# Two half-filled matmuls of the first layers issued as a pair on the two row halves of TensorE

## The reference

```python
# attention: batch 4, 8 heads, 768 steps, head size 40; q, k, v, three gates
for t in range(S):
    m_new = maximum(f[t] + m, i[t])
    C = exp(f[t] + m - m_new) * C + exp(i[t] - m_new) * outer(v[t], k[t])
    n = exp(f[t] + m - m_new) * n + exp(i[t] - m_new) * k[t]
    y[t] = sigmoid(o[t]) * (C @ q[t]) / maximum(abs(n . q[t]), 1)
x = y.transpose(0, 2, 1, 3).reshape(3072, 320)
# first MLP
h = x @ w_in            # 320 -> 2048
x = maximum(0.01 * h, h) @ w_out      # 2048 -> 320
# second MLP, weights of its own
h = x @ w2_in
out = (h * cos(h)) @ w2_out
```

## Time and profile before

| | |
|---|---|
| median of 3 executions | 838.56 us (837.67 to 840.02) |
| the profiled execution | 840.17 us, span 838.4 us |
| TensorE matmuls busy | 818.4 us, 98% of the span, 6939 matmuls |
| VectorE, ScalarE, GpSimd busy | 76%, 55%, 41% |
| mean granted TensorE clock | 0.989 of full speed |
| first MLP with attention of the next blocks | from about 37 us to 477 us |
| second MLP | from about 477 us to the end |

### The profile page before, as it was taken

The page is one execution under the profiler, slowest core; times in us unless marked ns, Lnnn a source line. Parts: engine busy times, 40 slices in busy tenths (PEclk is TensorE's granted clock), DMA queues, the critical chain, the costliest instruction groups (busy, mean ns, idle before and its releaser), DMA issues.

```text
span 838.4 us, 18237 instructions
## 1 busy us (share of the span) xinstructions
PE 818.4 (98%) x6939; PEld 787.9 (94%) x6939; DVE 636.8 (76%) x1377; ACT 465.1 (55%) x1033; POOL 339.6 (41%) x350
## 2 busy tenths in 40 slices
PE   8789999999999999999999999999999999999997
PEld 6679899999999999999999999999999999999997
DVE  7778678677677776777754488888888888888886
ACT  5245343433443434334436687767677767777776
POOL 5755634344333333443315643333333333333332
PEclk9989999999999999999999999999999999999999
DMA  8494433322334333226023320302020202020000
GB/s 262 130 249 129 151 84 93 125 78 80 125 104 128 124 81 125 78 78 194 2 90 100 106 102 2 118 2 72 1 72 1 72 1 71 1 72 1 17 8 25
DMA packets 37292, 70.26 MB, mean 84 GB/s; under 512 B 3544, under 2 KB 24408, under 8 KB 37208
## 3 DMA queue, kind: packets, MB, share of 16 engines
q1 hardware_dynamic: 36708, 68.86, 26.5%
q10 hardware_dynamic: 500, 0.26, 0.1%
HBM read 57.11 MB, written 11.99 MB: 82 GB/s over the span
## 4 chain that ended last, share of the span: by engine, by line
PE 90%; DVE 5%; ACT 2%; DMA 1%; issue 1%; SPq 1%; POOL 1%; DVEq 0%; POOLq 0%; ACTq 0%
PE h L621 31%; PE acc L633 13%; PE acc L635 13%; PE acc L634 12%; PE s L621 10%; PE x L599 2%; PE s L579 2%; PE s L563 2%; PE s L591 2%; PE s L544 1%; DMA raw_out<-w1o 1%; DVE g_lo L1180 1%; DVE C L1161 1%; DVE t_f L1037 1%; DMA e_dram<-r_f 0%
## 5 line engine op out<-in xcount | busy, mean ns | idle before, releaser
L621 PE MATMUL h<-xT,w_in 128*128 128x384 f32 x1536 | 307.8, 342 | 0.7 <-DVE xT L1172 0.7
L621 PEld LDWEIGHTS h<-xT,w_in 128*128 128x128 f32 x1536 | 267.8, 189 | 3.8 <-DVE xT L1172 0.9
L777 ACT ACTIVATE t_f<-h 128x384 f32<-128x384 f32 x192 | 94.1, 490 | 294.5 <-PE h L621 294.4
L633 PE MATMUL acc<-w_out,g_hi 128*128 128x320 f32 x768 | 242.7, 316 | 2.1 <-POOL g_lo L1519 1.7
L635 PE MATMUL acc<-w_out,g_lo 128*128 128x320 f32 x768 | 237.9, 310 | 0.0
L634 PE MATMUL acc<-w_out,g_hi 128*128 128x320 f32 x768 | 236.7, 308 | 0.0
L1519 POOL TENSOR_TENSOR g_lo<-g_f,g_hi 128x384 fp32r<-128x384 f32 x127 | 130.0, 1023 | 212.1 <-ACT g_hi L777 212.1
L1193 DVE TENSOR_TENSOR g_f<-h,t_f 128x384 f32<-128x384 f32 x128 | 71.2, 556 | 109.2 <-ACT t_f L777 109.1
L633 PEld LDWEIGHTS acc<-w_out,g_hi 128*128 128x128 f32 x768 | 144.9, 189 | 4.6 <-POOL g_lo L1519 1.9
L634 PEld LDWEIGHTS acc<-w_out,g_hi 128*128 128x128 f32 x768 | 145.1, 189 | 0.0
L635 PEld LDWEIGHTS acc<-w_out,g_lo 128*128 128x128 f32 x768 | 144.7, 188 | 0.0
(11 more groups left out here) (150 smaller groups left out, 797.6 us busy)
## 6 DMA issues: line engine op xcount, KB each, us to landing
qk_s<-qk SPq DMA_DIRECT2D x24, 512.0 KB, 3.8
kvo_s<-kvo SPq DMA_DIRECT2D x24, 484.0 KB, 5.2
x_dram<-stage SPq DMA_DIRECT2D x8, 960.0 KB, 5.5
xT<-x_dram SPq DMA_DIRECT2D x8, 960.0 KB, 4.9
D<-g_dram SPq DMA_DIRECT2D x42, 128.0 KB
qe<-q SPq DMA_DIRECT2D x24, 160.0 KB, 5.5
out<-x SPq DMA_DIRECT2D x24, 160.0 KB, 1.8
eG_b<-e_dram SPq DMA_DIRECT2D x42, 80.0 KB
```

The source lines that it names most:

```text
L621: last = nc.tensor.matmul(bank[:, 0:BLOCK], w(a), x[:, k, :], start=(n == 0), stop=(n == 7))
L633: nc.tensor.matmul(acc[t][:, 0:DM], g_hi[:, s, r], w_out[:, 0, j, :], start=(j == 0), stop=False)
L777: copy = lambda o, i, **k: nc.scalar.activation(o, i, ACT.Copy, **k)
```

## The change

`w_in` loses chunk 5. Chunk 2 now holds, for an even tile, the high part of the rest in rows 0 to 63 and its low part in rows 64 to 127; for an odd tile the two are swapped (`rest_rows`). `xT` and `stage` gain chunk 5: chunk 2 holds the rest's high part in both halves, chunk 5 its low part in both. Matmul (2, 2) gives high times high and low times high. What is left, high times low, has 64 rows. It is one matmul of 64 rows for each tile, on rows 0 to 63 for an even tile and on rows 64 to 127 for an odd one (`rest_product`). Both are issued behind the seven full ones of the even tile, one behind the other, into two banks. So an even slot has 7 full matmuls and the pair, an odd slot 7 full ones. The wait for the odd tile's bank moves from its slot into the even slot, ahead of the second of the pair. `split_turned` is one instruction of 128 x 384 instead of two. The low parts of the weights are written in two or three instructions instead of one, on GpSimd with a wait between them. The tokens' DRAM buffer grows from 5 to 6 chunks.

```diff
-        w_in = sb("w_in", [P, 6, FF], F32R)
+        w_in = sb("w_in", [P, 5, FF], F32R)
-        xT = sb("xT", [P, 2, 5, BLOCK], F32R)
-        stage_f = sb("stage", [P, 5, BLOCK])
+        xT = sb("xT", [P, 2, 6, BLOCK], F32R)
+        stage_f = sb("stage", [P, 6, BLOCK])
...
+        def rest_rows(j):
+            return slice(SUB * (1 - j % 2), SUB * (2 - j % 2))
...
             def first_product(bank, x, j):
                 w = lambda k: w_in[:, k, j * P:(j + 1) * P]
-                order = [(0, 0), (0, 3), (3, 0), (1, 1), (1, 4), (4, 1), (2, 2), (5, 2)]
+                order = [(0, 0), (0, 3), (3, 0), (1, 1), (1, 4), (4, 1), (2, 2)]
                 for n, (a, k) in enumerate(order):
-                    last = nc.tensor.matmul(bank[:, 0:BLOCK], w(a), x[:, k, :], start=(n == 0), stop=(n == 7))
+                    last = nc.tensor.matmul(bank[:, 0:BLOCK], w(a), x[:, k, :], start=(n == 0 and j % 2 == 0),
+                                            stop=(n == 6 and j % 2 == 1))
+                if j % 2 == 0:
+                    last = rest_product(bank, x, j)
                 last.then_inc(h_done, 1)
+
+            def rest_product(bank, x, j):
+                r = side(j % 2)
+                return nc.tensor.matmul(bank[:, 0:BLOCK], w_in[r, 2, j * P:(j + 1) * P], x[r, 5, :], start=(j % 2 == 1), stop=(j % 2 == 0))
...
-                    pe.wait_ge(max_done, row.tile(i) - 1 + H_FREE)
+                    if j % 2 == 0:
+                        pe.wait_ge(max_done, row.tile(i) - 1 + H_FREE)
                     first_product(h_bank[i % 2], xT[:, row.half(i)], j)
+                    if j % 2 == 0:
+                        pe.wait_ge(max_done, row.tile(i) + H_FREE)
+                        rest_product(h_bank[1], xT[:, row.half(i)], j + 1)
                 elif exists(row, i):
...
-                    pe.wait_ge(prod_done, row.tile2(i) - 3 + PROD_FREE)
+                    if j % 2 == 0:
...
+                        pe.wait_ge(prod_done, row.tile2(i) - 3 + PROD_FREE)
                     first_product(ring_bank[i % 4], xT[:, row.half(i)], j)
+                    if j % 2 == 0:
...
+                        pe.wait_ge(prod_done, row.tile2(i) - 2 + PROD_FREE)
+                        rest_product(ring_bank[(i + 1) % 4], xT[:, row.half(i)], j + 1)
...
-                tt(dst[:, 3:5, r], src[:, 0:2, :], dst[:, 0:2, r].bitcast(F32), ALU.subtract)
-                return tt(dst[REM:P, 2, r], src[REM:P, 2, :], dst[REM:P, 2, r].bitcast(F32), ALU.subtract)
+                return tt(dst[:, 3:6, r], src, dst[:, 0:3, r].bitcast(F32), ALU.subtract)
...
 (VectorE, six pieces of two tiles)
-                tt(w_in[:, 3:6, c], raw_in[:, k % RAW_IN, :, :], w_in[:, 0:3, c].bitcast(F32), ALU.subtract).then_inc(win_lo, 1)
+                for j in range(PT):
+                    r, b = rest_rows(j), slice((k * PT + j) * P, (k * PT + j + 1) * P)
+                    tt(w_in[r, 2, b], raw_in[r, k % RAW_IN, 2, j * P:(j + 1) * P], w_in[r, 2, b].bitcast(F32), ALU.subtract)
+                tt(w_in[:, 3:5, c], raw_in[:, k % RAW_IN, 0:2, :], w_in[:, 0:2, c].bitcast(F32), ALU.subtract).then_inc(win_lo, 1)
...
 (GpSimd, two pieces; the second MLP's tiles likewise, in two instructions)
-                nc.gpsimd.tensor_tensor(w_in[:, 3:6, c], raw_in[:, k % RAW_IN, :, :], w_in[:, 0:3, c].bitcast(F32),
-                                        ALU.subtract).then_inc(win_lo, 1)
+                nc.gpsimd.tensor_tensor(w_in[:, 3:5, c], raw_in[:, k % RAW_IN, 0:2, :], w_in[:, 0:2, c].bitcast(F32),
+                                        ALU.subtract).then_inc(win_step, 1)
+                pool.wait_ge(win_step, PT * k + 1)
+                for j in range(PT):
+                    r, b = rest_rows(j), slice((k * PT + j) * P, (k * PT + j + 1) * P)
+                    nc.gpsimd.tensor_tensor(w_in[r, 2, b], raw_in[r, k % RAW_IN, 2, j * P:(j + 1) * P], w_in[r, 2, b].bitcast(F32),
+                                            ALU.subtract).then_inc(win_step if j == 0 else win_lo, 1)
+                    if j == 0:
+                        pool.wait_ge(win_step, PT * k + 2)
...
-    x2_dram = nc.dram_tensor("x2_dram", [BLOCKS, P, 5, BLOCK], F32, kind="Internal").ap()
+    x2_dram = nc.dram_tensor("x2_dram", [BLOCKS, P, 6, BLOCK], F32, kind="Internal").ap()
```

More of the change, by code:

```diff
@@ L164, in build @@
         win_lo = sem("win_lo")
+        win_step = sem("win_step")
         wout_hi = sem("wout_hi")
@@ L661, in slot @@
                         pe.wait_ge(x2_in[row.half(i)], row.block(i) * 8 - 8 * row.half(i) - 48)
[L662 to L665, removed]
-                    pe.wait_ge(prod_done, row.tile2(i) - 3 + PROD_FREE)
-                    first_product(ring_bank[i % 4], xT[:, row.half(i)], j)
+                    if j % 2 == 0:
+                        if row.starts(BLOCKS, i):
+                            pe.wait_ge(win_lo, PIECES + j + 2)
+                            if j == 0:
+                                pe.wait_ge(max_done, row.tile(i) - 1 + H_FREE)
+                        pe.wait_ge(prod_done, row.tile2(i) - 3 + PROD_FREE)
+                    first_product(ring_bank[i % 4], xT[:, row.half(i)], j)
+                    if j % 2 == 0:
+                        if row.starts(BLOCKS, i) and j == 0:
+                            pe.wait_ge(max_done, row.tile(i) + H_FREE)
+                        pe.wait_ge(prod_done, row.tile2(i) - 2 + PROD_FREE)
+                        rest_product(ring_bank[(i + 1) % 4], xT[:, row.half(i)], j + 1)
                 if (u := row.unit(i, TURN)) and j < FT - 1:
@@ L1455, in swap_in_lo @@
                 k, c = PIECES + j // PT, slice(j * P, (j + 1) * P)
-                nc.gpsimd.tensor_tensor(w_in[:, 3:6, c], raw_in[:, k % RAW_IN, :, j % PT * P:(j % PT + 1) * P],
-                                        w_in[:, 0:3, c].bitcast(F32), ALU.subtract).then_inc(win_lo, 1)
+                r, b = rest_rows(j), slice(j % PT * P, (j % PT + 1) * P)
+                nc.gpsimd.tensor_tensor(w_in[:, 3:5, c], raw_in[:, k % RAW_IN, 0:2, b], w_in[:, 0:2, c].bitcast(F32),
+                                        ALU.subtract).then_inc(win_step, 1)
+                pool.wait_ge(win_step, PT * RAW_IN + j + 1)
+                nc.gpsimd.tensor_tensor(w_in[r, 2, c], raw_in[r, k % RAW_IN, 2, b], w_in[r, 2, c].bitcast(F32),
+                                        ALU.subtract).then_inc(win_lo, 1)
+                pool.wait_ge(win_lo, PIECES + j + 1)
             def swap_out_lo(j):
```

## The result

| | before | after |
|---|---|---|
| median of 4 runs each, same chip | 838.13 us (837.67 to 840.02) | 864.36 us (862.51 to 864.64) |
| ratio | | 1.0306, 95% interval 1.0285 to 1.0328 |
| the profiled execution | 840.17 us, span 838.4 | 864.11 us, span 862.4 |
| TensorE matmuls busy | 818.4 us | 840.1 us |
| VectorE busy | 636.8 us | 635.7 us |

The account below looks back on a forecast made before the run. TensorE was taken to bound the kernel, with 90% of the chain. Pairs' net +28.8 us, shared switches -2.4 and first block -0.5 gave +25.9 on 838.56, so 864.5 us; range 858 to 871, widened to 854 to 873.

Parts of the forecast that it names:

- The step that decides: TensorE entering and leaving the 64-row shape costs 0.40 us a pair, against 0.175 gained by running side by side.
- Rivals 1 to 3: Shape change free or cheap (816 us if free, chance 0.06); half price (0.09); pair not side by side (887 us, 0.05).
- rival 2: Half the switch price, for instance if entry's cost hangs on a semaphore wait: 842 or 839 us; chance 0.09.
- What the profile was to show: Second MLP: two slots 5.68 us, entry 0.27, second layer's first matmul 0.35; TensorE 90% or more; VectorE's busy time falls.
- The net of a pair: Switch cost less matmul time saved: +0.225 us for each of 128 pairs, +28.8 us.
- The shared switch: Blocks 1 to 6, slots 0 and 10: scores follow, so the pair adds one shape change, 12 times 0.20, -2.4 us.
- The moved waits: Waits for the odd tile's bank, moved forward, cost nothing: 1.25 us to spare in first MLP, 2.5 in second.
- VectorE's and GpSimd's edits: Weight splits and units' low parts: hidden, priced at nothing; uncovered, up to 2 us in the first block.
- DMA: Tokens' buffer a fifth larger: landings of at most 6.6 and 5.9 us, loaded a block ahead, cost nothing.
- The forecast's own range: 858 to 871 us for switches of 0.36 to 0.45 us a pair, chance 0.80; widened to 854 to 873.
- the first block's bounds: First block's 8 pairs: -0.5 us taken for hidden ones, bounds -1.8 (all hidden) and +3 (low clock, other edits showing).
- The total: Whole kernel: +28.8 - 2.4 - 0.5 = +25.9 us, median to 864.5 us, 3.1% slower.

Follow-up runs that it names:

- e3: Changed kernel without the pair's second matmul (odd tiles lack high times low of the rest), waits as before the change: 864.76 us, ratio 1.0311.
- e4: Changed kernel with both matmuls of the pair on rows 0 to 63: 884.56 us, ratio 1.0534.
- e1: Changed kernel with its other edits, but one full 128-row matmul per tile instead of the pair and waits where they were: 842.91 us, ratio 1.0032.
- e8: e1 with 93 tiles of the second MLP run wholly in 64-row halves, both layers, upper halves not added up: 839.72 us, ratio 0.9994.
- e6: Changed kernel with 80 instead of 128 stationary columns in both matmuls of the pair: 858.14 us, ratio 1.022.
- e2: e1 with the eighth matmul of odd tiles left out, so 15 full matmuls for two tiles and no pair: 822.22 us, ratio 0.9801.
- e5: e1 with 18 pairs only, in blocks 1 to 6, straight behind the state unit: 840.48 us, ratio 1.0013.
- e7: Changed kernel with 64 instead of 384 moving columns in both matmuls of the pair: 848.61 us, ratio 1.0099.
- v1: Kernel before, with the low part of the rest in six first-block weight pieces moved from VectorE to GpSimd: 841.45 us, ratio 1.003.
- e10: e1 without the twelve small VectorE instructions writing the rest's low part for the first MLP's tiles 4 to 15: 834.93 us, ratio 0.9959.

## Why the prediction was right, point by point

**The step that decides: right.** Forecast: 0.09 at entry, 0.11 for the pair's first load, 0.09 and 0.11 at the exit. Found: 0.095 ahead of the pair, 0.194 between it and the second layer (its load and the drain), 0.104 ahead of that layer's second matmul (its first load); 0.396 against 0.40. That it runs side by side: e3 and e4. That it is the shape and nothing else: e1 at 0.00 in steady blocks, and e8 paying 0.38 to 0.41 where full and halved layers meet. That the load is in the open: e6. Rivals 1 to 3 are out; rival 2 since the entry has its gap though the pair's first matmul waits for no semaphore.

**What the profile was to show.** 5.68 us for two slots (5.66), 0.27 (0.27), a duration longer by 0.11 (0.44 against 0.34), 0.35 for the second layer's first matmul (0.34). Two signs were off: TensorE has 88% of the chain and not 90% or more, and VectorE's busy time fell by 1.1 us where I had 4 to 5. The units' low parts gave their 7 us and the weights' took 3 more than before. Most of the rest is a subtraction that the change doesn't touch, that of `g_lo`, before and after:

```profile
L1180 DVE TENSOR_TENSOR g_lo<-g_f,g_hi 128x384 fp32r<-128x384 f32 x128 | 95.3, 744 | 0.0
```

```profile
L1202 DVE TENSOR_TENSOR g_lo<-g_f,g_hi 128x384 fp32r<-128x384 f32 x128 | 100.1, 782 | 0.0
```

Its 128 instructions took 4.8 us more, and the longest 4.2 us where it was 1.7.

**The net of a pair: 0.225 forecast, 0.204 found.** The 0.40 fits, but seven full matmuls lost small delays that eight had: the odd slots became shorter by 0.197 in the second MLP and not by 0.175. In blocks 1 to 6 many of them became shorter by 0.173 only, and there the pair costs 0.23. Why the pace of 384 columns wavers between 0.173 and 0.185 is open.

**The shared switch: right.** In slots 0 and 10 of the blocks with attention the even slot grew by 0.20 instead of 0.404, twelve times. The chain of such a slot, with the scores (L549) behind the pair:

```profile
330.99 0.37 PE h L635
331.36 0.63 PE s L549 x32
331.99 0.35 PE acc L646
```

Scores took 0.62 before and the second layer 0.35 behind them: the change back was paid there already.

**Missed: two waits in blocks 1 and 6.** One slot in each grew by 0.87 us that no pair explains. The chain in block 1, then the timeline with it:

```profile
135.05 1.55 DVE g_lo L1202
...
136.80 0.47 DVE x L1158 x2
137.27 0.04 issue
137.31 0.55 PE x L604 x3
```

```profile
134.89 1.29 POOL L1367 TENSOR_TENSOR D<-D,hide 128x512 f32<-128x512 f32 x1
134.97 1.63 DVE L1202 TENSOR_TENSOR g_lo<-g_f,g_hi 128x384 fp32r<-128x384 f32 x1
```

VectorE's subtraction, 0.55 us as a rule, started 0.08 us behind GpSimd's mask and lasted 1.63; the transposes came late. In the kernel before the same two started in the other order at this place, and there the mask took 1.57 us. These are odd slots, which become shorter elsewhere; here the two grew by 0.67 and 0.68 us. In the other kernels with longer slots the same two grew too, by 0.66 and 0.69 in e3, 0.70 and 0.72 in e6, 0.48 and 0.51 in e4. In e1, e2, e5 and e7, whose pairs of slots are 0.09 us longer at most, they didn't. So the waits come with the longer slots, which shift the other engines' work against GpSimd's; that last step is argued from the two orders and was not tried by itself. The Trainium skill, "SBUF — State Buffer", section "SBUF: two separate sides", says that a VectorE instruction with two SBUF inputs and a GpSimd instruction that reads SBUF need one port pair, which the first to start holds for its whole length. These rows agree (VectorE's ended 0.42 us behind the mask), and so do the two of L1293 shown above, each of which ended 0.15 us behind GpSimd's.

**The moved waits: right.** TensorE waited for L1215 behind the pair once, 0.2 us, and ahead of a first layer once, 0.4, in the whole span. The second of these e1 has too, where nothing was moved.

**VectorE's and GpSimd's edits: priced at nothing, about 3 us in e1.** This step failed, at the end of its stated bound (+3 for the first block). I sized the small instruction at its solitary 0.29; its mean was 0.675. A unit's low parts in one instruction (0.52 to 0.55 us for 0.68) did shorten five blocks' last slots by 0.17 each, where TensorE's transposes had waited for them.

**DMA: as said.** These answer to the earlier trace rows, and nobody waits:

```profile
x_dram<-stage SPq DMA_DIRECT2D x8, 1152.0 KB, 6.6
xT<-x_dram SPq DMA_DIRECT2D x8, 1152.0 KB, 5.1
```

**A slip in the range.** The forecast's own range was said to be 858 to 871 us with the first block's bounds. Its lower end has them; the upper end doesn't. With 0.45 us a pair and +3 for the first block the sum is 874, outside even the widened 873. The result is far from that end, so nothing hung on it.

**The total.** The two profiled executions differ by 23.9 us (their spans by 24.0), where the sum had 25.9. By blocks, from the starts of the first layers: the first block and what is ahead of it +1.3, the six blocks with attention behind it +8.6, the other nine +14.2. The nine have 72 pairs at 0.204, 14.7, and gain 0.5 at the start of the second MLP. The six have 48 pairs at 0.204 (9.8), the shared switches (-2.4), the single instruction (-0.9) and the two waits (+1.7), which makes 8.2; the 0.4 left are uneven slots (odd ones that give back 0.17, slots with transposes that grow by 0.35). The first block's 1.3 can't be divided: e1 has +3.9 there without pairs, and the clock differs from run to run. The profile of before was 2.0 us above its median and that of after 0.3 below: 26.2 us between the medians. So that 864.36 lies so near to 864.5 owes something to luck: the sum was 2.0 us too high, and the 1.6 us that I took off, since the profiled run of before lay above its median, had no counterpart in the run of after.

## What to carry to other kernels

Price a change of matmul shape by the round trip, not by the work saved: here 0.40 us, more than two full matmuls of 384 columns, and two half-filled ones in parallel save one. Look for a place where the array is in that shape already (0.21 for the pair behind the state unit, and a gain), or stay in it. On VectorE and GpSimd, count instructions that meet on the two engines, not columns: one more small one can cost the length of the neighbour's, fewer columns can take more time (v1), and a later slot can turn around who waits.

## What the runs showed of the hardware that was not expected

- 64-row halves on both sides keep the full pace for whole blocks (0.175 us for two matmuls of 384 columns with their loads, e8).
- A VectorE subtraction of 64 x 128 took up to 2.81 us beside GpSimd, and 0.29 alone. One of 128 x 512 (0.68 alone) took 4.71 while GpSimd ran four instructions one behind the other (v1): it didn't get its turn between them.
- A full matmul removed from a steady series gave 0.173 us in e2 (0.02 in the one slot in eight that then waited for ScalarE) and 0.197 in the odd slots of the changed kernel, against a pace of 0.175.
- From 28 to 101 us the granted clock had means of 0.88 to 0.98 in kernels that do nearly the same. 6.4 us less of VectorE's work (e10 against e1) went with a clock of 0.98 instead of 0.91 there and with 6 to 8 us less time.
